# Split-row router logits and a re-ordered routing stage in a fused attention, expert and MLP kernel

## What is computed

```python
# 1. windowed attention: 4 batches, 8 heads, 576 positions, head size 64
x = attention(q, k, v).transpose(0, 2, 1, 3).reshape(2304, 512)
# 2. one expert of 8 per row
xn = x / (norm(x) + 1e-6);  en = emb / (norm(emb) + 1e-6)
logits = xn @ en.T / tau                      # 2304 x 8
e = argmax(logits, 1);  gate = softmax(logits)[e]
out[row] = gate * (relu(x[row] @ w1[e]) @ w2[e])      # 512 -> 1024 -> 512
# 3. an MLP on every row
h = out @ w_in;  y = (h * cos(h)) @ w_out             # 512 -> 2048 -> 512
```

## Time and profile before

| | us |
|---|---|
| median of 3 runs | 864.06 |
| lowest, highest of them | 863.76, 866.65 |
| profiled execution, its own time | 867.19 |
| span of its trace | 865.2 |
| PE busy | 832.7 (96%) |
| DVE busy | 604.9 (70%) |
| ACT busy | 481.7 (56%) |
| POOL busy | 75.9 (9%) |

### The profile page before, as it was taken

One profiled execution on the slowest core, in us unless ns is written; L12 is line 12 of the kernel. 1 busy time (PEld: TensorE's weight loads), 2 busy tenths in 40 slices (PEclk: granted clock), 3 DMA queues, 4 the chain that ended last, 5 costly groups with the idle time before them and its releaser, 6 DMA issues.

```text
span 865.2 us, 15473 instructions
## 1 busy us (share of the span) xinstructions
PE 832.7 (96%) x5034; PEld 756.8 (87%) x5034; DVE 604.9 (70%) x1162; ACT 481.7 (56%) x921; POOL 75.9 (9%) x129
## 2 busy tenths in 40 slices
PE   7999999969999999999999999999999999999994
PEld 5888786669999999999998999998999998999993
DVE  6888986575555555455567777788777788777762
ACT  4566765315545555444466666676656667656652
POOL 3112112141001000000000000002000003000002
PEclk9999999999999999999999999999999999999998
DMA  6597886134445433443432121113212213121001
GB/s 147 121 222 178 198 190 198 44 110 158 129 161 174 142 126 123 146 144 125 140 106 74 49 73 61 63 69 127 73 50 73 67 56 146 50 73 53 22 1 73
DMA packets 114912, 93.78 MB, mean 108 GB/s; under 512 B 65816, under 2 KB 94488, under 8 KB 114848
## 3 DMA queue, kind: packets, MB, share of 16 engines
q1 hardware_dynamic: 109920, 78.81, 31.5%
q0 software_dynamic: 4928, 14.16, 4.9%
HBM read 83.51 MB, written 9.44 MB: 107 GB/s over the span
## 4 chain that ended last, share of the span: by engine, by line
PE 84%; DVE 7%; issue 2%; ACT 2%; DMA 2%; POOL 1%; another core or an unknown queue 0%; DVEq 0%; ACTq 0%; POOLq 0%; SPq 0%
PE bank L721 24%; PE bank L719 24%; PE bank L720 24%; PE bank L607 2%; PE bank L586 2%; PE bank L660 2%; PE bank L595 1%; PE bank L570 1%; DVE shifted L1195 1%; DVE row_max L1192 1%; ACT probs L898 1%; PE bank L676 1%; DMA xtok<-x_rows 1%; DVE kT L319 1%; PE bank L761 1%
## 5 line engine op out<-in xcount | busy, mean ns | idle before, releaser
L719 PE MATMUL bank<-yh,up_l 128*128 128x384 f32 x384 | 129.5, 337 | 0.5 <-DVE yl L1486 0.5
L721 PE MATMUL bank<-yh,up_h 128*128 128x384 f32 x384 | 129.5, 337 | 0.0
L720 PE MATMUL bank<-yl,up_h 128*128 128x384 f32 x384 | 129.0, 336 | 0.0
L721 PE MATMUL bank<-dn_h,hid 128*128 128x512 f32 x288 | 113.9, 396 | 0.0
L719 PE MATMUL bank<-dn_h,hid 128*128 128x512 f32 x288 | 112.5, 391 | 1.4 <-DVE hid L1464 1.4
L720 PE MATMUL bank<-dn_l,hid 128*128 128x512 f32 x288 | 113.7, 395 | 0.0
L1254 DVE TENSOR_TENSOR dn_l<-dn_raw,dn_h 128x512 fp32r<-128x512 f32 (+1 forms) x79 | 71.8, 909 | 56.3 <-ACT dn_h L949 52.2
L1067 ACT ACTIVATE work<-bank 128x384 f32<-128x384 f32 x96 | 47.2, 492 | 79.6 <-PE bank L721 78.8
L719 PE MATMUL bank<-xh,up_l 128*128 128x352 f32 x256 | 84.6, 330 | 4.7 <-DVE xl L1386 3.3
L949 ACT ACTIVATE dn_h<-dn_raw 128x512 fp32r<-128x512 f32 (+1 forms) x79 | 63.7, 806 | 41.5 <-PE bank L721 41.5
L1079 ACT ACTIVATE work<-work 128x384 f32<-128x384 f32 x96 | 50.5, 526 | 63.9 <-DVE work L1459 61.1
(11 more groups left out here) (197 smaller groups left out, 1685.6 us busy)
## 6 DMA issues: line engine op xcount, KB each, us to landing
up_raw<-in_moe_w_dram SPq DMA_DIRECT2D x32, 512.0 KB, 3.5
dn_raw<-in_moe_w_dram SPq DMA_DIRECT2D x32, 512.0 KB, 3.6
up_raw<-in_moe_w_in_dram SPq DMA_DIRECT2D x24, 512.0 KB, 3.4
dn_raw<-in_moe_w_out_dram SPq DMA_DIRECT2D x24, 512.0 KB, 3.5
qn<-in_q_dram SPq DMA_DIRECT2D x32, 144.0 KB, 2.7
kn<-in_k_dram SPq DMA_DIRECT2D x32, 144.0 KB, 3.1
xtok<-x_rows SPq DMA_DIRECT2D x4, 1152.0 KB, 7.5
x_rows<-osb POOLq DMA_DIRECT2D x8, 288.0 KB, 3.5
```

Of the source, the lines that this page charges most:

```text
L719: mm(o, w[1], x[0], start=first, stop=False, skip_group_check=True)
L720: mm(o, w[0], x[1], start=False, stop=False, skip_group_check=True)
L721: return mm(o, w[0], x[0], start=False, stop=last, skip_group_check=True)
```

## The change

1. **Split-row logits.** ACT makes the high part `xTh` of all transposed rows, DVE the low part `xTl` (in place of a copy each). `embT` holds high and low columns, 16 in all, in fp32r. PE multiplies 4 blocks of `xTh` and 4 of `xTl` with it. ACT copies the 16 x 192 result, PE turns it at once (`turn`, two transposes a round) and DVE adds the two parts (`join`).
2. **Norms.** ACT squares four of the last tiles behind the rounds, DVE two (`square_sums`).
3. **Routing chain.** The counts come out of PE in expert order, so their copy goes. ACT makes one of the two parts of `to_row` and a quarter of `in_lane`. The division by the norm and the exponentials move behind the masks, and `id_now` moves ahead of the sum of exponentials. Fewer fills.
4. **Second weights of expert 0** are split before the block: `up` ahead of the lane masks on ACT and behind the gates on DVE, `dn` behind the exponentials on ACT and behind the first tiles on DVE.
5. **Table** instructions L1358 to L1364 move behind the first three tiles. DVE's wait for the table and its reads of it move behind block 0.
6. **First three units** are begun on the 128 rows of tile 0, and `expert_up` then does the other 224.

```diff
@@ PE @@
             def logits(G):
-                pe.wait_ge(xt_out_a, G + 1)
-                pe.wait_ge(xt_out_d, G + 1)
+                pe.wait_ge(xt_hi, 2 * G + 2)
                 if G >= 2:
                     pe.wait_ge(lt_out, G - 1)
                 for d in range(DT):
-                    last = mm(bank[4 + G % 2][:E, 0:2 * QT], embT[:, d, :], xT[G % 2][:, d, :], start=d == 0, stop=d == DT - 1)
+                    mm(bank[4 + G % 2][:2 * E, 0:2 * QT], embT[:, d, :], xTh[G % 2][:, d, :],
+                       start=d == 0, stop=False, skip_group_check=True)
+                pe.wait_ge(xt_lo, 2 * G + 2)
+                for d in range(DT):
+                    last = mm(bank[4 + G % 2][:2 * E, 0:2 * QT], embT[:, d, :], xTl[G % 2][:, d, :],
+                              start=False, stop=d == DT - 1, skip_group_check=True)
                 last.then_inc(lt_done, 1)
+            def turn(G):
+                pe.wait_ge(lt_out, G + 1)
+                if G >= 2:
+                    pe.wait_ge(joined, G - 1)
+                for t in range(2):
+                    last = tp(bank[6 + G % 2][:QT, t * 2 * E:(t + 1) * 2 * E], logT[:, (2 * G + t) * QT:(2 * G + t + 1) * QT], ident[:2 * E, :2 * E])
+                last.then_inc(turned, 1)
...
+                if G >= 2:
+                    turn(G - 2)
             logits(RT // 2 - 1)
-            for t in range(RT):
-                last = tp(bank[7][:QT, t * E:(t + 1) * E], logT[:, t * QT:(t + 1) * QT], ident[:E, :E])
+            turn(RT // 2 - 2)
+            turn(RT // 2 - 1)
...
-            fill(24)
+            fill(19)
+            pe.wait_ge(row_part, 1)
+            for n, t in enumerate((*tiles[:-2 * LANE_TILES], *tiles[-LANE_TILES:], *tiles[-2 * LANE_TILES:-LANE_TILES])):
...
-            fill(14)
+            fill(9)
...
-            fill(3)
+            fill(2)
+            def first_tile_up(f):
+                pe.wait_ge(ex["up_lo"], f // 2 + 3)
+                pe.wait_ge(ex["in_lo"], FIRST_INC[0])
+                cols = slice(f % 2 * P, f % 2 * P + P)
+                s = f // 2
+                for d in range(DT):
+                    passes(bank[4 + f][:, 0:P], (up_h[s][:, d, cols], up_l[s][:, d, cols]),
+                           (xh[0][:, d, 0:P], xl[0][:, d, 0:P]), d == 0, d == DT - 1)
             def expert_up(i, u, f):
+                first_col = P if isinstance(i, int) and 2 * i + u == 0 and f < EARLY_UNITS else 0
...
-            for tile in range(3):
-                transpose_rows(tile, tile)
-                fill((8, 1, 3)[tile])
+            transpose_rows(0, 0)
+            fill(2)
+            transpose_rows(1, 1)
+            first_tile_up(0)
+            transpose_rows(2, 2)
+            for f in range(1, EARLY_UNITS):
+                first_tile_up(f)
             expert_block(0, 0)
@@ ACT @@
+            logits_out(RT // 2 - 1)
+            for t in range(NT - 2):
+                squares(B, t)
+            expert_up_hi(0, 1)
+            act.wait_ge(lane_nums, 1)
+            for t in range(LANE_TILES):
+                last = A(lane_sq[:, t, :], lane_no[:], ACT.Square, scale=-1.0, bias=lane_f[:, RT - LANE_TILES + t:RT - LANE_TILES + t + 1])
+            last.then_inc(lane_sq_ready, 1)
+            act.wait_ge(in_tile_ready, 1)
+            A(to_row[:, :, 0, :], in_tile[:], ACT.Copy, scale=row_no[:, 0:1]).then_inc(row_part, 1)
+            act.wait_ge(lane_sq_ready, 1)
+            A(in_lane[:, RT - LANE_TILES:, :], lane_sq[:], ACT.Relu, scale=-1.0, bias=one_f[:QT, 0:1]).then_inc(lanes_act, 1)
             act.wait_ge(shifted_ready, 1)
             A(lg[:, 3, :, :], lg[:, 2, :, :], ACT.Exp).then_inc(row_exp, 1)
+            expert_dn_hi(0, 1)
@@ DVE @@
             for G in range(RT // 2):
-                cp(xT[G % 2][:, 2:4, :], bank[2 * (G % 2) + 1][:, 0:4 * QT].rearrange("p (d c) -> p d c", d=2)).then_inc(xt_out_d, 1)
-                if G >= 1:
-                    logits_out(G - 1)
+                for j in range(2):
+                    dve.wait_ge(xt_hi, 2 * G + j + 1)
+                    tt(xTl[G % 2][:, 2 * j:2 * j + 2, :], bank[2 * (G % 2) + j][:, 0:4 * QT].rearrange("p (d c) -> p d c", d=2),
+                       xTh[G % 2][:, 2 * j:2 * j + 2, :], ALU.subtract).then_inc(xt_lo, 1)
+                if G >= 2:
+                    join(G - 2)
...
+                if G >= RT // 2 - 2:
+                    square_sums(RT - RT // 2 + G)
...
-            link(cp(tile_rows[:, 1:].rearrange("p (e t) -> p e t", e=E), bank[5][:, RT * E:2 * RT * E].rearrange("p (t e) -> p e t", t=RT)))
-            link(V.tensor_tensor_scan(base[:], running[:], tile_rows[:], 0.0, ALU.mult, ALU.add))
+            link(V.tensor_tensor_scan(base[:, 1:], running[:, 1:], bank[5][:, RT * E:2 * RT * E], 0.0, ALU.mult, ALU.add))
...
+            cp(lane_f[:], place[:, 1, :]).then_inc(lane_nums, 1)
...
-            ts(to_row[:, :, 0, :], in_tile[:], row_no[:, 0:1], None, ALU.mult)
-            for t0 in range(0, RT, LANE_TILES):
+            for t0 in range(0, RT - LANE_TILES, LANE_TILES):
...
+            dve.wait_ge(row_ids_done, 1)
+            link(cp(gates[:], bank[6][:, 0:ST]))
+            tt(id_now[:], gates[:], bank[6][:, ST:2 * ST], ALU.add).then_inc(ids_ready, 1)
...
             V.tensor_reduce(gates[:], bank[7][:, 0:3 * ST].rearrange("p (a c) -> p c a", a=3), AX_X, ALU.add).then_inc(gates_ready, 1)
+            expert_up_lo(0, 1)
+            for tile in range(3):
+                first_rows_lo(tile)
+            for tile in range(3):
+                tile_rows_out(tile, tile)
+            expert_dn_lo(0, 1)
             link(V.tensor_tensor_scan(row(cum_blocks), one_f[:], row(blocks), 0.0, ALU.mult, ALU.add))
...
-            dve.wait_ge(table_ready, 1)
+            expert_block(0, 0, None)
             nblk = dve.value_load(table[0:1, 2, 0:1], min_val=SURE, max_val=NBLK)
```

More of the change, by code:

```diff
@@ L118, in fused_kernel @@
         xtok = sb1("xtok", [QT, RT, DM])
-        xT = [sb1(f"xT{i}", [P, DT, 2 * QT]) for i in range(2)]
-        logT = sb1("logT", [E, N])
+        xTh = [sb1(f"xTh{i}", [P, DT, 2 * QT], F32R) for i in range(2)]
+        xTl = [sb1(f"xTl{i}", [P, DT, 2 * QT], F32R) for i in range(2)]
+        logT = sb1("logT", [2 * E, N])
+        logit = sb1("logit", [QT, RT, E])
+        sq_junk_d = sb1("sq_junk_d", [QT, DM])
         emb_sb = sb1("emb_sb", [E, DM])
@@ L734, in expert_up @@
                 for d in range(DT):
-                    last = passes(bank[4 + f % 4][:, 0:TB], (up_h[s][:, d, cols], up_l[s][:, d, cols]),
-                                  (xh[u][:, d, :], xl[u][:, d, :]), d == 0, d == DT - 1)
+                    last = passes(bank[4 + f % 4][:, first_col:TB], (up_h[s][:, d, cols], up_l[s][:, d, cols]),
+                                  (xh[u][:, d, first_col:], xl[u][:, d, first_col:]), d == 0, d == DT - 1)
                 last.then_inc(ex["up_mm"], 1)
@@ L1030, in expert_block @@
                     if f < FT - 2:
-                        (expert_up_hi, expert_dn_hi)[f % 2](i, J)
+                        if not (sure and b == 0 and f < 2):
+                            (expert_up_hi, expert_dn_hi)[f % 2](i, J)
                     elif f == FT - 2:
@@ L1287, in _, with over_tiles @@
             tt(onehot[:], lg[:, 1, :, :], over_e(small[:, 1, :]), ALU.is_equal).then_inc(onehot_ready, 1)
+            dve.wait_ge(onehot_ready, 1)
+            dve.wait_ge(counts_done, 1)
+            link(V.tensor_tensor_scan(base[:, 1:], running[:, 1:], bank[5][:, RT * E:2 * RT * E], 0.0, ALU.mult, ALU.add))
+            link(tt(lg[:, 4, :, :], bank[5][:QT, 0:RT * E].rearrange("p (t e) -> p t e", t=RT),
+                    base[:QT, 0:E * RT].rearrange("p (e t) -> p t e", e=E), ALU.add))
+            link(tt(lg[:, 1, :, :], lg[:, 4, :, :], onehot[:], ALU.mult))
+            link(V.tensor_reduce(small[:, 6, :], lg[:, 1, :, :], AX_X, ALU.add))
+            link(cp(place[:, 0, :], small[:, 6, :]))
+            ts(place[:, 1, :], place[:, 0, :], P - 1, None, ALU.bitwise_and)
+            link(ts(place[:, 2, :], place[:, 0, :], 7, None, ALU.arith_shift_right))
+            cp(lane_f[:], place[:, 1, :]).then_inc(lane_nums, 1)
+            def over_tiles(x):
+                return x.unsqueeze(2).broadcast_to([QT, RT, ST])
+            tt(in_tile[:], over_tiles(place[:, 2, :]), tile_no[:].unsqueeze(1).broadcast_to([QT, RT, ST]),
+               ALU.is_equal).then_inc(in_tile_ready, 1)
+            dve.wait_ge(in_tile_ready, 1)
+            tt(to_row[:, :, 1, :], in_tile[:], over_tiles(first_no[:]), ALU.mult)
+            for t0 in range(0, RT - LANE_TILES, LANE_TILES):
+                tiles = slice(t0, t0 + LANE_TILES)
+                tt(in_lane[:, tiles, :], place[:, 1, tiles].unsqueeze(2).broadcast_to([QT, LANE_TILES, P]),
+                   lane_no[:].unsqueeze(1).broadcast_to([QT, LANE_TILES, P]), ALU.is_equal).then_inc(lanes_ready, 1)
             dve.wait_ge(root_ready, 1)
@@ L1411, in expert_block @@
                     if f == 5:
```

(5 more changed lines are left out.)

120 lines of the change are left out of this document (62 added, 58 removed).

## The result

| | before | after |
|---|---|---|
| median, us (8 runs each, taken together) | 866.28 | 859.92 |
| lowest, highest | 863.76, 871.19 | 857.78, 863.01 |
| ratio after / before, 95% interval | | 0.9922 [0.9902, 0.9942] |
| profiled execution, its own time | 867.19 | 860.01 |
| span of its trace | 865.2 | 858.1 |

A forecast was written before the change was run, and what follows sets the result against it. PE is full from 200 us, so an earlier first second-half product moves the end. Median 864.06 - 4.0 (logits) - (4.5 - 2.75) + 0.3 (attention loop) + 0.5 (clock) = 859.1; forecast 859.3, range 855.0 to 864.0.

The forecast's parts named there:

- Logits stage: Twelve PE rounds shorten from 2.21 to 1.64 us; stage 24.2 instead of 28.2, gain 4.0, bounds 2.5 to 5.0.
- Rival, short passes at a plain f32 pace: Short fp32r passes in logits stage and first units don't run at one column a cycle: 892 us; chance 0.12.
- Rival, the clock falls in the logits stage: Fewer products per round lower PE's clock there; stage 40 us instead of 28, 874 in all; chance 0.04.
- Rival, ACT or DVE as the bound of the rounds: Both 0.4 us a round over the count, or remote wait in every execution: 862 us; joint chance 0.08.
- Row numbers: Routing chain on DVE: earlier scan 0.65, work taken off 1.03, earlier `id_now` 0.55; row numbers 2.2 us earlier.
- The gates: Behind the row numbers in the routing chain, with the 1.26 us exponentials' sum after them: 0.9 us earlier, at 182.0.
- `xl`: Low parts of the first three tiles, complete at 188.0 us instead of 191.2; 2.75 of this is the remote wait.
- What is late next: Before the first second-half product PE waits about 2.3 us for DVE's `hid`, behind `XS`, `dn` weights and table; product at 195.8.
- The stall for the second weights: PE's wait of 1.38 us up to 198.48, ahead of the first second-half product, goes.
- The clock: A fall between masks and 185 us or in the wait for DVE, in half the executions, worth 1 to 1.7; 0.5 taken.
- The remote wait: ACT's 2.75 us wait before copying tile 1, taken as an event of some executions that the median doesn't hold.

The follow-up runs named there:

- f_route: Changed kernel with routing-stage fills of 24, 16 and 5 instead of 19, 9 and 2; 860.27 us, ratio 0.9906 to the kernel before.
- tr2_first: Changed kernel with the transposes of tile 2 ahead of early unit 0; 857.42 us, ratio 0.987 to the kernel before.
- t_table: Changed kernel with the table's instructions moved behind the low parts of `hid` of units 0 and 1 on DVE; 855.83 us, ratio 0.9875 to the kernel before.
- a_again: The changed kernel run again, unchanged; 862.82 us, ratio 0.991 to the kernel before.
- b_again: The kernel before, unchanged, profiled a second time in one execution; 867.22 us.
- u_early: Changed kernel without early units, the first three units running whole on 352 rows; 859.1 us, ratio 0.9868 to the kernel before.
- both: Changed kernel with the table behind the low parts of `hid` and no early units; 858.85 us, ratio 0.9889 to the kernel before.
- f_gap: Changed kernel with eight fill products ahead of the first `dn_l` product; 859.04 us, ratio 0.9915 to the kernel before.

## Why the prediction was right or wrong

I forecast 859.3 us, and 7.7 less than the profiled execution before; it is 859.92, and 7.2 less. The direction, the range and most of the order were right. Step by step:

- **Logits stage: right mechanism, wrong size.** Gain 4.0 forecast, 5.0 my upper bound, 6.2 measured. The short passes behave as forecast: eight take 0.72. The turn takes 0.19 for my 0.11 (within its bounds), so twelve rounds are 20.6 and not 19.7. But the stage lasts 22.0, which leaves 1.4 for all that I put at 4.5 (1.2 for weight splits, 2.7 for start and tail, 0.6 for waits). The failed terms are these. The weight splits, two on ACT and two on DVE, don't hold up PE: the chain is PE's alone from 141.94 to 157.34, and of these 15.40 us DVE is busy 12.36 and ACT 11.92. PE's waits for `xTl` add up to 0.4. And the products and turn of the last round stood in my sum twice, in the twelfth round and in the tail, which is 3.2 from 157.34 to 160.54 and holds them.
- **Rival, short passes at a plain f32 pace: refuted** by 0.09 us a pass. The early passes of 128 columns and the shortened ones of 224 both start 0.11 us apart. This agrees with the rule of the Trainium skill that I weighed ("TensorE: Matmul & The Clock Gate", section LDWEIGHTS (loading the stationary operand)), by which a load takes its columns / 1.2 GHz, 107 ns for 128. The price of this rival was wrong by its own terms: 12 rounds of 3.7 and 2.7 of start and tail are 47.1 us, 18.9 more than 28.2 and not 15.
- **Rival, the clock falls in the logits stage: refuted.** It is 1.00 at 140 to 145 and over the 15.40 us of the rounds, with 0.72 of each 1.72 us in products. The Trainium skill (same page, "Part 4: PE-mode transpose") has transposes not count as products do; in every trace here the clock stayed at 1.00 through this stage, so nothing here shows it or speaks against it.
- **Rival, ACT or DVE as the bound of the rounds: refuted** by the same 15.40 us, in which PE never waits.
- **Row numbers: 2.2 forecast, 1.6 measured.** Two costs were set at nothing that weren't. From the first count product to the scan I gained 0.39 and not 0.65, as the strided product lasts twice as long; my bound of 0.2 for it was 0.06 short. And "needed only behind the masks, 9 us later" was no reason to leave POOL's norms out: the masks themselves slow POOL, the norms end 9.7 us behind the start of the row maximum, and the division waits 0.55. The gates gained 0.7 for 0.9.
- **`xl`: 3.2 forecast, 1.8 measured.** From the gates on I had 5.8 us; 6.2 is the value at full clock (f_route) and the low stretch adds 0.9. What made the 0.4 isn't shown. Early unit 0 was in my sum, with 1.3 us ahead of tile 2, and that was right; what I did not ask is whether it should stand there. It holds up tile 2, and with it DVE's whole chain, by 1.5 us, as tr2_first shows.
- **What is late next: right.** Forecast was a wait of 2.3 for DVE's `hid` behind `XS`, `dn_l` and the table, 7.8 from `xl` to the product; it is 2.11, and 7.55. t_table confirms the cause. The stall for the second weights is gone as said.
- **The clock: the cost was too low.** I took 0.5 for all of it, from falls worth 1 to 1.7 in half of the executions. The profile after has two that cost: 0.9 around tile 1 and 2.3 behind the wait. A fall behind a wait of over 2 us for `hid` is in four of the five profiles that have one (not in a_again); there is one behind the waits of 1.87 and 2.92 for `up_l` too, and none behind those of 0.31 and 0.76 for `hid`. In these stretches second-half passes start 0.29 us apart instead of 0.16.
- **The remote wait: right as an event, wrong in its price.** I left its 2.75 us out of the median, since the first three runs had a median of 864.06. The wait is in fact missing in another execution, but that one took 867.22 (b_again), as much as the one with it: PE waits 2.9 for `up_l` where it waited 1.38, its low clock only comes later, and its first transposes started 1.0 later. Counted from those, the wait was worth 0.8 us. The median of the kernel before was 866.28 over the first eight runs and 867.53 to 870.05 in the three sets beside the experiments. The level that I started from was lower than all of these, and that, with the missing 2.2 in the logits stage on one side and the clock and `xl` on the other, is why the time came out so near. The nearness, 859.3 for 859.92, is luck: against the median the forecast gain was 4.8 us and the measured one 6.4.

By parts: split-row logits carry the gain. Early second weights exchange one wait for another. The early units gain nothing in this place, and the first of them holds up tile 2; without them the product comes earlier (by 0.8 in u_early, by 1.5 in the run `both`) and the end does not. The order of the work that DVE does, or waits for, behind the first tiles gives 3 to 4 us more once changed: t_table and tr2_first reach 0.9875 and 0.987 of the kernel before. These two and u_early can't be told from each other. The two orders together, t_table with tr2_first, were not run.

Two things stay open. From the first second-half product to the end four traces of the kernel after and its variants take 664.7 to 664.8 us at full clock, but tr2_first and u_early 665.5 and the run `both` 666.1. The difference lies in the expert blocks (246.0 to 247.4 us up to the first product of the MLP, and 418.7 to 418.8 from there in t_table, f_gap, tr2_first, u_early and `both`), and the waits of PE behind the product, 2.7 to 2.8 us in all, are the same in each. And the first transposes start up to 4 us apart in kernels with the same attention stage, so differences of 1 to 2 us between medians of so few executions are not to be trusted where the traces don't show them.

## What to carry to other kernels

When an engine is given work early to fill a gap, look at what stands behind that work in its queue and who waits for that: here 1.5 us of early products held back the one tile on which the late engine's chain hung. When a stall is removed, write down the next engine's whole queue up to the same event; if something in it is needed only later, as the table here, move it in the same change. And don't add a share for every split that lies beside a full PE: with DVE busy 80% and ACT 77% of the rounds none of them reached PE.

## What the runs showed of the hardware

- Small POOL instructions on 96 x 24 values take 0.20 to 0.34 us with no masks beside them and 0.57 to 0.83 while DVE and ACT make the 16-bit masks (96 x 432 and 96 x 768); the fifteen took 7.15 us, and 4.6 once the masks were out of the way. DVE's masks are enough for it, as two slow steps have no mask instruction of ACT beside them; ACT's f32 squares alone did not slow POOL.
- A bf16 product of 192 columns whose moving operand is read with a stride lasted 0.50; its neighbour without one 0.24, and the same product without a stride in the kernel before 0.24.
- The low clock comes in stretches of 3 to 20 us whose place and number change from one execution of the same kernel to the next (171 to 174, 178 to 181 and 191 to 195 in one profile of the kernel after, 172 to 182 in the other). By the traces they move an execution by up to 3 us; of the six executions of a_again the four at a mean clock of 0.983 took 2 to 5 us more than the two at 0.990 and 0.993.
